# Delta-rule attention ahead of two expert stages: outputs formed transposed in column tiles, states in two tiles, loads issued by SyncE

## The reference, cut to what matters

```
y[t]  = q[t] . state                               # per batch (4) and head (8), state is 48 x 48
state = state + beta[t] * outer(kn[t], v[t] - state^T . kn[t])      # 768 steps t, kn = k / (|k| + 1e-6)
x = y as 3072 tokens x 384
h = x @ w_in; x = (h * tanh(softplus(h))) @ w_out  # 384 -> 2048 -> 384
P = softmax-like gate, 8 rounds of row and column scaling; out = sum over 8 experts of P[e] * (relu(x @ w1[e]) @ w2[e])
```

## Time and profile before

| | us |
|---|---|
| median of 3 runs (2446.39 to 2450.2) | 2447.94 |
| the profiled execution | 2450.1 |
| its span, first to last instruction | 2448.3 |

### The profile page before, as it was taken

The page is one execution under the profiler, slowest core; times in us unless marked ns, Lnnn a source line. Parts: engine busy times, 40 slices in busy tenths (PEclk is TensorE's granted clock), DMA queues, the critical chain, the costliest instruction groups (busy, mean ns, idle before and its releaser), DMA issues.

```text
span 2448.3 us, 37209 instructions
## 1 busy us (share of the span) xinstructions
PE 2407.9 (98%) x15256; PEld 2024.2 (83%) x15256; DVE 1292.9 (53%) x2413; ACT 873.7 (36%) x1900; POOL 425.1 (17%) x344
## 2 busy tenths in 40 slices
PE   6999999999999999999999999999999999999999
PEld 5888888888888878888888888888888888888887
DVE  4787777697777746333333333333333333333344
ACT  5777878676666621111111111111111111111111
POOL 6676676100000000000000000000000000000000
PEclk8999999999999999999999999999999999999999
DMA  1110110120000010110110101101101011011013
GB/s 63 45 45 24 45 46 30 34 58 1 0 0 0 27 34 14 41 43 9 48 43 14 48 18 40 43 9 48 43 14 48 18 39 43 9 48 44 18 30 70
DMA packets 59020, 79.05 MB, mean 32 GB/s; under 512 B 37600, under 2 KB 38368, under 8 KB 56928
## 3 DMA queue, kind: packets, MB, share of 16 engines
q1 hardware_dynamic: 54400, 63.33, 8.4%
q10 hardware_dynamic: 4464, 13.50, 1.6%
HBM read 71.81 MB, written 5.01 MB: 31 GB/s over the span
## 4 chain that ended last, share of the span: by engine, by line
PE 91%; DVE 4%; ACT 2%; POOL 1%; issue 1%; ACTq 0%; DMA 0%; DVEq 0%; SPq 0%; POOLq 0%
PE ex_y L55 45%; PE ex_h L55 44%; ACT at_Z L360 1%; PE ex_y L537 1%; DVE at_gram L445 1%; PE ex_logits L55 1%; ACT at_T L362 1%; DVE at_X L408 1%; DVE de_w_lo L766 0%; DVE de_hg L794 0%; DVE de_en L781 0%; DVE de_g_lo L774 0%; ACT at_X L347 0%; DVE de_en L779 0%; POOL at_RT L339 0%
## 5 line engine op out<-in xcount | busy, mean ns | idle before, releaser
L1215 DVE SCALAR_TENSOR_TENSOR ex_r_lo<-ex_h,ex_r_hi 128x512 fp32r<-128x512 f32 x384 | 265.0, 690 | 929.2 <-ACT ex_r_hi L1094 928.8
L1094 ACT ACTIVATE ex_r_hi<-ex_h 128x512 fp32r<-128x512 f32 x384 | 230.1, 599 | 1284.5 <-PE ex_h L55 1284.4
L55 PE MATMUL ex_h<-x_hi,ex_w_lo 128*128 128x512 f32 x1152 | 448.1, 389 | 0.0
L55 PE MATMUL ex_h<-x_lo,ex_w_hi 128*128 128x512 f32 x1152 | 448.1, 389 | 0.0
L55 PE MATMUL ex_h<-x_hi,ex_w_hi 128*128 128x512 f32 x1152 | 448.1, 389 | 0.0
L55 PE MATMUL ex_y<-ex_r_hi,ex_w_lo 128*128 128x512 f32 x1152 | 448.1, 389 | 0.0
L55 PE MATMUL ex_y<-ex_r_hi,ex_w_hi 128*128 128x512 f32 x1152 | 448.1, 389 | 0.0
L55 PE MATMUL ex_y<-ex_r_lo,ex_w_hi 128*128 128x512 f32 x1152 | 448.1, 389 | 0.0
L1044 POOL TENSOR_TENSOR ex_w_lo<-ex_stage,ex_w_hi 128x512 fp32r<-128x512 f32 x90 | 115.9, 1288 | 1691.6 <-ACT ex_w_hi L1076 1653.4
L55 PEld LDWEIGHTS ex_y<-ex_r_hi,ex_w_lo 128*128 128x128 f32 x1152 | 216.2, 188 | 45.0
L55 PEld LDWEIGHTS ex_h<-x_hi,ex_w_hi 128*128 128x128 f32 x1152 | 216.2, 188 | 45.1 <-issue 0.2
(11 more groups left out here) (150 smaller groups left out, 3333.1 us busy)
## 6 DMA issues: line engine op xcount, KB each, us to landing
ex_stage<-w_exp SPq DMA_DIRECT2D x15, 1536.0 KB, 6.6
ex_pb<-p_rows SPq DMA_DIRECT2D x90, 256.0 KB, 3.4
at_qT<-q_t ACTq DMA_DIRECT2D x10, 512.0 KB, 4.1
at_v_in<-v ACTq DMA_DIRECT2D x11, 384.0 KB, 3.1
at_k_in<-k ACTq DMA_DIRECT2D x10, 384.0 KB, 4.8
out<-ex_stage SPq DMA_DIRECT2D x60, 64.0 KB, 1.9
de_stage<-w_in SPq DMA_DIRECT2D x8, 384.0 KB, 3.3
de_stage<-w_out SPq DMA_DIRECT2D x8, 384.0 KB, 3.2
```

What stands on the lines that cost most here:

```text
L55: return nc.tensor.matmul(out, lhsT, rhs, start=start, stop=stop)
L1094: nc.scalar.activation(r[0][:, j, :], h_bank[j][:], ACT.Relu).then_inc(hi_ready, 1)
L1215: nc.vector.scalar_tensor_tensor(out=r[1][:, j, :], in0=h_bank[j][:], scalar=0.0, in1=r[0][:, j, :].bitcast(F32), op0=ALU.max, op1=ALU.sub ...
```

## The change

- **Outputs.** Y, B3 and B5 go, and the query half of B1. In their place stand Q.u and W.u, for the two halves u of a wave. Q multiplies the old state by the queries, W multiplies U by the query part of `gram`, both with the state or U as the stationary operand, so that the output arises transposed, 32 head dimensions at a time, in one of four column tiles of the array (PSUM partitions 0, 32, 64, 96). Per half that is 12 + 16 full-precision matmuls of 32 (four of them 16) stationary and 128 moving columns. The rows of x then have another order: the first 32 dimensions of the eight heads fill two blocks of 128, the last 16 of each the third. U has gaps of zeros between heads for that, and for odd heads the two parts of v are swapped.
- **States.** B4 writes two column tiles of 64 (4 matmuls per group, 48 moving columns) where it wrote the full width (2 matmuls, 96 columns).
- **First chunk.** B1 and Q are left out where the state is zero; R is then a copy of the scaled v.
- **Loads.** SyncE issues k, v and q of all rounds. v comes in three transfers of 48, 32 and 16 floats a row. In the start's order k of round 1 now stands ahead of v.
- **Order.** Each engine has a list of its own for a round, by step and group (`ATTENTION_ROUND`), with `@+1` for the next round and `@-1` for the one before. On GpSimd bv is ahead of kn also in round 0. The banks are set by `ATTENTION_BANKS`.
- **Unit columns.** From the second merge on only half as many are copied.
- **w_in.** Since the rows of x have another order, the rows of w_in must have it too. SyncE loads each w_in piece by 17 transfers, one for each run of `output_rows`, of 16 or 32 partitions with 2 x 512 bytes on each; w_out stays at one.

```
-DENSE_WEIGHTS = {("X", 1): -3, ("Z", 5): -2, "res": -1}
-ATTENTION_TAIL = ([("B2", g) for g in range(4)] + [("h", 0), ("B3", 0), ("B3", 1), ("h", 1), ("g", 0), ("B3", 2), ("B3", 3),
-                                                   ("g", 1), ("B5", 0), ("B5", 1)])
+ATTENTION_ROUND = {
+    "PE": (
+        "H.0 H.1 H.2 H.3 B2.0@-1 X0.0 X0.1 X0.2 X0.3 B2.1@-1 T0.0 T0.1 T0.2 T0.3 B2.2@-1 Z0.0 Z0.1 Z0.2 Z0.3 "
+        "B2.3@-1 X1.0 X1.1 X1.2 X1.3 Q.0@-1 W.0@-1 T1.0 T1.1 T1.2 T1.3 B4.0@-1 B4.1@-1 Z1.0 Z1.1 Z1.2 Z1.3 "
+        "Q.1@-1 W.1@-1 X2.0 X2.1 X2.2 X2.3 B4.2@-1 B4.3@-1 T2.0 T2.1 T2.2 T2.3 Z2.0 Z2.1 Z2.2 Z2.3 X3.0 X3.1 "
+        "X3.2 X3.3 T3.0 T3.1 T3.2 T3.3 F1.0@+1 F1.1@+1 Z3.0 Z3.1 Z3.2 Z3.3 F2.0@+1 X4.0 X4.1 X4.2 X4.3 F1.2@+1 "
+        "F2.1@+1 T4.0 T4.1 T4.2 T4.3 F1.3@+1 Z4.0 Z4.1 Z4.2 Z4.3 F2.2@+1 X5.0 X5.1 X5.2 X5.3 F2.3@+1 T5.0 T5.1 "
+        "T5.2 T5.3 B1.0 Z5.0 Z5.1 Z5.2 Z5.3 B1.1 res.0 res.1 res.2 res.3 B1.2 corr.0 corr.1 corr.2 corr.3 B1.3 "),
+    "ACT": (
+        "eH.0 eH.1 eH.2 eH.3 u0.0 u0.1 u0.2 u0.3 sqrt@+1 eT0.0 eT0.1 eT0.2 eT0.3 eZ0.0 eZ0.1 eZ0.2 eZ0.3 u1.0 "
+        "u1.1 u1.2 u1.3 xhi.0@-1 eT1.0 eT1.1 eT1.2 eT1.3 eZ1.0 eZ1.1 eZ1.2 eZ1.3 xhi.1@-1 u2.0 u2.1 u2.2 u2.3 "
+        "eT2.0 eT2.1 eT2.2 eT2.3 eZ2.0 eZ2.1 eZ2.2 eZ2.3 u3.0 u3.1 u3.2 u3.3 eT3.0 eT3.1 eT3.2 eT3.3 eF1.0@+1 "
+        "eF1.1@+1 eZ3.0 eZ3.1 eZ3.2 eZ3.3 u4.0 u4.1 u4.2 u4.3 eF1.2@+1 eT4.0 eT4.1 eT4.2 eT4.3 eF1.3@+1 eZ4.0 "
+        "eZ4.1 eZ4.2 eZ4.3 u5.0 u5.1 u5.2 u5.3 eT5.0 eT5.1 eT5.2 eT5.3 eZ5.1 eZ5.3 eres.1 eres.3 "),
+    "DVE": (
+        "red@+1 U.0@-1 eX0.0 eX0.1 eX0.2 eX0.3 U.1@-1 inv@+1 U.2@-1 U.3@-1 eX1.0 eX1.1 eX1.2 eX1.3 xlo.0@-1 "
+        "st.0@-1 st.1@-1 xlo.1@-1 eX2.0 eX2.1 eX2.2 eX2.3 st.2@-1 st.3@-1 eX3.0 eX3.1 eX3.2 eX3.3 gram.0@+1 "
+        "gram.1@+1 eX4.0 eX4.1 eX4.2 eX4.3 gram.2@+1 gram.3@+1 gram.4@+1 gram.5@+1 eX5.0 eX5.1 eX5.2 eX5.3 "
+        "gram.6@+1 gram.7@+1 R.0 eZ5.0 eZ5.2 R.1 eres.0 eres.2 R.2 ecorr.0 ecorr.1 ecorr.2 ecorr.3 R.3 "),
+    "POOL": (
+        "sq@+1 RT.0 RT.1 RT.2 RT.3 bk@+1 bv@+1 kn@+1 NT.0@+1 ZZ.0@+1 NT.1@+1 ZZ.1@+1 NT.2@+1 ZZ.2@+1 NT.3@+1 "
+        "ZZ.3@+1 "),
+    "SP": (
+        "loadk@+2 loadv@+1 q@+1 "),
+}
+ATTENTION_BANKS = {"B1.0": "0", "B1.1": "2", "B1.2": "0", "B1.3": "2", "B2.0": "1", "B2.1": "3", "B2.2": "1",
+                   "B2.3": "3", "B4.0": "1", "B4.1": "3", "B4.2": "1", "B4.3": "3", "F1.0": "0", "F1.1": "2",
+                   "F1.2": "0", "F1.3": "2", "F2.0": "01", "F2.1": "23", "F2.2": "01", "F2.3": "23", "Q.0": "0",
+                   "Q.1": "2"}
+ATTENTION_TAIL = {"PE": "B2.0 B2.1 B2.2 B2.3 Q.0 Q.1 W.0 W.1", "ACT": "xhi.0 xhi.1", "DVE": "U.0 U.1 U.2 U.3 xlo.0 xlo.1", "POOL": "", "SP": ""}
+ATTENTION_FILLS = {
+    "PE": {('W', 0, 11): [(0, 'h')], 'end': [(1, 'h')]},
+    "ACT": {('xhi', 0, 10): [(-3, '')], ('eres', 1, 10): [(-2, '')], ('eres', 3, 10): [(-1, '')], ('xhi', 0, 11): [(0, 'g')], 'end': [(1, 'g')]},
+    "DVE": {('eX1', 0, 11): [(-2, 'split')], ('eX2', 0, 11): [(-1, 'split')], ('xlo', 0, 11): [(0, 'g')], 'end': [(1, 'g')]},
+}
...
+    def load_v(eng, n):
+
+        to, rows = [x.rearrange("p (a b) d -> p a b d", b=2) for x in (v_in[:], v[n // W, n % W])]
+        eng.dma_start(to[:, :, 0, :], rows[:, :, 0, :]).then_inc(loaded_v, 16)
+        eng.dma_start(to[:, :, 1, D2:D], rows[:, :, 1, 0:D1]).then_inc(loaded_v, 16)
+        eng.dma_start(to[:, :, 1, 0:D2], rows[:, :, 1, D1:D]).then_inc(loaded_v, 16)
...
+    def sp_program(sp):
+        load_k(sp, 0)
+        sp.dma_start(beta_t[:], beta).then_inc(beta_in, 16)
+        load_k(sp, 1)
+        load_v(sp, 0)
+        sp.dma_start(mask[:], masks).then_inc(masks_in, 16)
+        load_q(sp, 0)
+        load_q(sp, 1)
+        for kind, g, n in steps("SP"):
+            if kind == "loadv" and n > 0:
+                sp.wait_ge(v_scaled, n)
+                load_v(sp, n)
+            if kind == "q" and n >= W:
+                for u in range(2):
+                    filled(sp, "Q", u, n - W)
+                load_q(sp, n)
+            if kind == "loadk" and n >= W:
+                sp.wait_ge(scaled, n - W + 1)
+                load_k(sp, n)
...
+            if kind == "bv":
+                if n == 0:
+                    pool.wait_ge(beta_in, 16)
+                pool.wait_ge(loaded_v, 48 * (n + 1))
...
+            elif kind[0] == "u":
+                i = int(kind[1:])
+                if i == 0:
+                    if n > 0:
+                        act.wait_ge(M_filled[g], m_count(n - 1, "corr"))
+                    else:
+                        act.wait_ge(ident_ready, 1)
+                to, units = pair_half(i, True, X[g]), pair_half(i, True, four(ident_h[:]))
+                if i:
+                    to, units = to[:, :, :, 0:MERGES[i] // 2], units[:, :, :, 0:MERGES[i] // 2]
+                nc.scalar.copy(to, units)
...
+            elif kind == "B1":
+                if not first_chunk(n):
+                    bank_free(pe, "B1", g, n)
+                    drained(pe, "F1", g, n)
+                    drained(pe, "B4", g, n - W)
+                    i = o_bank("B1", g)
+                    for a in range(2):
+                        last = mm(nc, O_bank[i][:, 2 * D * a:2 * D * (a + 1)], kbT[g][:, 2 * w, a, :],
+                                  state[:, w * H + 2 * g + a, :])
+                    last.then_inc(O_filled[i], 1)
...
+            elif kind == "Q":
+                bank_free(pe, "Q", g, n)
+                if not first_chunk(n):
+                    for x in (2 * g, 2 * g + 1):
+                        drained(pe, "B4", x, n - W)
+                    y = O_bank[o_bank("Q", g)][:, 0:MC * P].rearrange("p (m t) -> p m t", m=MC)
+                    old = state[:, w * H + 4 * g:w * H + 4 * g + 4, :]
+                    for m in range(2):
+                        for x in range(4):
+                            a, b = divmod(4 * m + x, 2)
+                            mm(nc, y[32 * x:32 * x + 32, m, :], old[:, a, D * b + D2 * b:D * b + D2 * b + D1], qT[w][:, 4 * g + a, :],
+                               start=(m == 0), stop=False)
+                    for a in range(4):
+                        mm(nc, y[32 * a:32 * a + 32, 2, :], old[:, a, D1:D1 + 2 * D2], qT[w][:, 4 * g + a, :], start=False, stop=False)
+            elif kind == "W":
+                for x in (2 * g, 2 * g + 1):
+                    drained(pe, "B2", x, n)
+                y = O_bank[o_bank("Q", g)][:, 0:MC * P].rearrange("p (m t) -> p m t", m=MC)
+
+                def attn(j):
+                    a, b = divmod(j % 4, 2)
+                    return gram[w][2 * g + j // 4][:, b, 1, a, :]
+
+                def u_cols(j, first, last):
+                    at = DP * (j % 4)
+                    return U[2 * g + j // 4][:].rearrange("p j e -> p (j e)")[:, at + first:at + last]
+
+                for m in range(2):
+                    for x in range(4):
+                        j = 4 * m + x
+                        mm(nc, y[32 * x:32 * x + 32, m, :], u_cols(j, D2 * (j % 2), D2 * (j % 2) + D1), attn(j),
+                           start=(m == 0 and first_chunk(n)), stop=False)
+                for a in range(4):
+                    j = 2 * a + 1
+                    mm(nc, y[32 * a:32 * a + 32, 2, :], u_cols(j, -D2, D2), attn(j), start=False, stop=False)
+                for a in range(4):
+                    j = 2 * a
+                    last = mm(nc, y[32 * a:32 * a + D2, 2, :], u_cols(j, D1, D), attn(j), start=False, stop=True)
+                last.then_inc(O_filled[o_bank("Q", g)], 1)
+            elif kind == "B4":
+                if not last_chunk(n):
+                    bank_free(pe, "B4", g, n)
+                    drained(pe, "B2", g, n)
+                    i = o_bank("B4", g)
+                    for a in range(2):
+                        for b in range(2):
+                            j = 2 * a + b
+                            last = mm(nc, O_bank[i][DP * b:DP * (b + 1), a * D:(a + 1) * D], kn[w][:, 4 * g + j, :],
+                                      U[g][:, j, 0:D])
+                    last.then_inc(O_filled[i], 1)
...
+def output_rows(H, D):
+
+
+    out = []
+    for h in range(H):
+        for first, size, m, at in ((0, 32, h // 4, 32 * (h % 4)), (32, D - 32, 2, (D - 32) * h)):
+            row = h * D + first
+            while size:
+                n = min(size, P - row % P)
+                out.append((m, at, row // P, row % P, n))
+                row, at, size = row + n, at + n, size - n
+    return out
...
+        for read in attention.inputs_read:
+            sp.wait_ge(*read)
         for n, (t, i) in enumerate(pieces):
             if n >= 2:
                 sp.wait_ge(wlo_ready, n - 1)
-            sp.dma_start(stage[n % 2][:], (w_in, w_out)[t][:, i * PIECE * CH:(i + 1) * PIECE * CH]).then_inc(staged[n % 2], 16)
+            if t == 1:
+                sp.dma_start(stage[n % 2][:], w_out[:, i * PIECE * CH:(i + 1) * PIECE * CH]).then_inc(staged[n % 2], 16)
```

(58 more changed lines are left out.)

586 lines of the change are left out of this document (250 added, 336 removed).

## The result

| | before | changed |
|---|---|---|
| median of the runs, us | 2448.47 | 2480.75 |
| the runs | 2446.39 to 2450.2 | 2464.49, 2470.98, 2480.75, 2481.69, 2482.68 |
| profiled execution, its span | 2450.1, 2448.3 | 2464.49, 2462.7 |
| mean granted clock of the profiled run | 0.995 | 0.991 |

The ratio is 1.0113, with a 95% interval from 1.0079 to 1.0147: the changed kernel is slower, by 32 us in the medians. Its runs lie 18 us apart, with granted clocks of 0.991 down to 0.983, and the profiled one is the fastest of them. So the trace shows 14.4 us of the 32.3; for the rest there are only the spans and mean clocks of the other runs.

What follows compares the result with a forecast made beforehand. TensorE, busy 98% of the span, was taken as the bound; rounds 0, start +2, first rounds and tail -3, w_in +19 and +8 gave +26, so 2474 us; range over all 2440 to 2500, the forecast's own 2452 to 2500.

Steps and rivals of the forecast that it cites:

- The rounds: Attention's 11 rounds: TensorE work -1.6 and waits +1.7 us a round, rounded to 0; bounds -1.5 and +2 a round.
- Q and W: TensorE in each round: 112 added instructions take 4.0 us, nearer to four column tiles at once, plus 0.4 for tile changes.
- B4: TensorE's state sums in each round: 1.8 us before, 2.1 after with changes of tile shape, +0.3.
- The waits: Merge steps and H in each round: +1.2 bare steps, +0.5 xlo, +0.4 corr sums, +0.1 elsewhere, 0.5 given back; +1.7 us.
- The start: Before TensorE's first work: bv stands ahead of kn and v lands later, near 9.3; +2 us, bounds 1.5 and 5.
- -3: B1 and Q of rounds 0 and 1 gone, and less in the tail before the dense steps: -3 us, bounds 0 and -6.
- w_in in the dense stage: First token block: 17 transfers at 0.52 us make a loop of 12.1 us where two pieces took 8.06; +19 us.
- w_in in attention: Last round: 34 issues land pieces 0 and 1 late, ScalarE's copy delays `eres.3` and H.3 by 7.1 us; +8 us.
- The clock: TensorE after the last round's pause: first matmuls slower, as at the start; 0.9 us, within the attention w_in term.
- Rival 1: Rounds give back all removed work, four column tiles at once: -3.1 us a round, 2440 us; chance 0.18.
- Rival 2: SyncE's issuing is cheap, 0.2 us a transfer, so w_in pieces land in time: no change, 2447 us; chance 0.12.
- rival 3: Column tiles of Q and W run one at a time: 88 us more over 11 rounds, 2562 us; chance 0.06.

Runs made afterwards that it cites:

- experiment 1: The changed kernel with w_in's rows laid out by the host, so that each w_in piece is one transfer: 2442.29 us, ratio 0.9979.
- experiment 2: The kernel before, with each w_in piece in 17 transfers and the order of the rows untouched: 2482.19 us, ratio 1.0137.
- experiment 10: The kernel of experiment 5 with B4 formed at full width again, one group after the other: 2437.25 us.
- Experiment 6: The kernel of experiment 1 with Q, W and B4 spread over gaps between merge steps and xhi, xlo later: 2435.14 us, ratio 0.9943.
- experiment 12: w_in laid out by the host, Experiment 6's order, experiment 5's kept work; kn ahead of bv in the first round: 2425.37 us, 2426.98 without this last edit.
- experiment 5: The kernel of experiment 1 with B1 and Q done also in the first chunk, where the state is zero: 2438.95 us, ratio 0.9953.
- experiment 3: The kernel of experiment 1 with 17 transfers again for w_in pieces 2 and on: 2464.87 us, ratio 1.0045.
- experiment 4: The kernel of experiment 1 with 17 transfers again for w_in pieces 0 and 1 only: 2458.77 us, ratio 1.0036.
- experiment 11: The changed kernel, w_in still in 17 transfers, with the work of the first chunk kept: 2472.93 us, ratio 1.0097.

## Why the prediction was right, and where it was not

The forecast was 2474 us and slower; 2480.75 came, inside the range. The cause it named, the 17 transfers of a w_in piece, is shown by experiments 1 and 2. That the number came within 7 us is luck: the sum was 11.6 us too high for the profiled execution (2474.3 against a span of 2462.7), most of it from the rounds, and the median lies 16 us above that execution, which no term of the sum foresaw.

- **The rounds** were put at 0 and are -0.86 a round, -9.5 over 11: the largest error of the sum. Work fell by 3.6 where I had 1.6. *Q and W* take 3.3 us (0.68 + 0.98, twice) where I took 4.4 with the tile changes. Q's 24 instructions in 0.68 are 0.028 each, a quarter of the 0.11 of one 128-column instruction: four tiles at once with nearly nothing lost. The Trainium skill, TensorE: Matmul & The Clock Gate, Part 3, led to an estimate of 3.8 from its three-tile figure; the trace, with four tiles, is below that. *B4* takes 1.2 where I took 2.1, but experiment 10 shows that in this order none of that reaches the round.
- **The waits** were put at +1.7 a round and are about +2.8 (3.6 less 0.86). The timelines say where. From T2 to the end of T3 it is 1.2, as forecast. H takes 1.04 longer than before, where I had 0.4 for the sums of `corr`. From X1 to T2 (290.13 to 296.07 before, 284.69 to 292.59 now) it is 1.96 longer with 0.9 more work, so about 1.1, where I had 0.6 for `xlo` and `xhi`. Given back from there to X1 (6.20 before, 5.63 now) are 0.57, as forecast (0.5). Experiment 6 wins back 1.05 by order alone.
- **A price that came out by luck.** The stretch from T2 to the end of T3 is 3.95 and I had 4.0, but my 3.49 for three bare steps came from 452.05 to 455.54, where the granted clock was 0.50 to 0.52. At full clock three of them take 2.98 (292.59 to 295.57) and the fourth 0.97 instead of my 0.5; the two errors cancel.
- **The start** was put at +2 and is +1.6 (10.43 to 12.00), but v was not late: bv found it there. Only bv standing ahead of kn costs, and experiment 12 takes 1.5 of it back. The *-3* for the first rounds and the tail is about -1: the first three intervals are 1.5 shorter than three rounds account for, and the tail has grown by 0.5. In other runs the work left out cost time instead, through the clock (experiment 5).
- **w_in in the dense stage** was put at +19. The mechanism is the one seen; the stage grew by 14.6 against the kernel before and by 16.0 against experiment 1 (421.27 us against 405.32). The loop took 10.9 to 11.6 us where I had 12.1, because in it the issue took 0.46 to 0.50 (I had 0.52) and the landing 1.7 (I had 1.9).
- **w_in in attention** was put at +8, and the last interval grew by 7.8 against the kernel before, 8.6 without the round's own gain; in experiment 2, with nothing else changed, by 8.1. The mechanism is the one seen, `eres` behind ScalarE's copy, but for both pieces. Against experiment 1 the pause is 11.05, and the 2.4 between the two is a gain that I overlooked: the kernel before had VectorE's splits of pieces 0 and 1 in this interval, which for that reason took 39.01 and not 36.55, and the new lists put them into the last round, behind `eX1` and `eX2`. The gain is read from the traces and was not tried by itself. These are rows of the kernel before, of VectorE and of TensorE:

```profile
425.97 1.68 DVE L766 TENSOR_TENSOR de_w_lo<-de_stage,de_w_hi 128x768 fp32r<-128x768 f32 x1 [0.36 <-ACT de_w_hi L708]
...
428.84 1.22 PE L55 MATMUL ex_h<-at_Z,at_X 128*128 128x128 f16 x16 [1.35 <-DVE at_X L413]
```

- **The two w_in terms together** were 27; they measure 26.9 against experiment 1 and 23.2 against the kernel before, which is what the sum was taken from.
- **The clock** was left out of the sum except for 0.9. After a pause, or after a thin stretch in rounds 1 and 2, TensorE ran at the lower of its two levels for a few to over 25 us. That this lifts the median 16 us above the profiled run is argued from the mean clocks of the upper runs (0.983 to 0.985 against 0.991) and the profiled runs of experiments 2, 3, 4 and 11; there is no trace of a run at 2482 of the changed kernel.

Rival 1 (a round shorter by more than 2.8 us) was right that the tiles run four at once and wrong that the drains keep up. Rival 2 fell with the first row of SyncE, rival 3 with the first row of Q.

## What to carry to other kernels

Count transfers, not bytes, when a layout changes: a buffer reloaded in a loop pays the issue of each of them, here 16 x 0.46 us, on the path as soon as the loop's slack is used up; a new row order is best made where the array is laid out. Where an engine copies a loaded piece in order ahead of a drain, ask how far ahead of that drain the issue starts. Work that is removed between dependent steps comes back as waits unless the rest is spread over the gaps, one piece in each, and where useless matmuls have been left out, look at the granted clock in that stretch, in more than one run.
